# Loading the experts' rows from another queue, and reordering the end of the attention stage, in a fused attention, expert and feed-forward kernel

## What is computed

```python
# 1. linear attention: B, H, S, D = 2, 8, 768, 48
for t in range(S):
    kt, vt, rt = k[:, :, t], v[:, :, t], r[:, :, t]
    cur = einsum('bhd,bhe->bhde', u[None] * kt, vt)
    y[:, :, t] = einsum('bhd,bhde->bhe', rt, state + cur)
    state = w[None, :, :, None] * state + einsum('bhd,bhe->bhde', kt, vt)
# 2. experts: 1536 tokens of 384, 8 experts with 1024 hidden, at most 384 tokens each
logits = x @ w_gate                 # the best expert of each token
probs = softmax(logits)             # its probability weighs the result
h = maximum(disp @ w1[e], 0)        # disp: the expert's tokens, in order
out[i] = gate_w[i] * (h @ w2[e])[pos[i]]
# 3. feed-forward: 384 -> 2048 -> 384
h = x @ w_in
out = (h * clip(h + 3, 0, 6) / 6) @ w_out
```

## Time and profile before

| | |
|---|---|
| median of 3 runs | 525.84 us (524.63 to 528.38) |
| profiled execution | 524.35 us, its span 522.6 us |
| PE busy | 442.9 us, 85% of the span |
| DVE, ACT, POOL busy | 243.1, 209.2, 73.2 us |
| TensorE's granted clock, mean | 0.927 of full speed |
| transfers | 60.55 MB, mean 116 GB/s |

### The profile page before, as it was taken

One profiled execution on the slowest core, in us unless ns is written; L12 is line 12 of the kernel. 1 busy time (PEld: TensorE's weight loads), 2 busy tenths in 40 slices (PEclk: granted clock), 3 DMA queues, 4 the chain that ended last, 5 costly groups with the idle time before them and its releaser, 6 DMA issues.

```text
span 522.6 us, 7372 instructions
## 1 busy us (share of the span) xinstructions
PE 442.9 (85%) x2798; PEld 380.3 (73%) x2798; DVE 243.1 (47%) x491; ACT 209.2 (40%) x481; POOL 73.2 (14%) x85
## 2 busy tenths in 40 slices
PE   6878998894776839494949989999999999999994
PEld 3767887673776839494949867888878888788883
DVE  6837885642736336262718556222522333332222
ACT  2433677350615235252526465223433323422221
POOL 4727761301010101010101010000000000000000
PEclk9777999999696969698898999999999999999999
DMA  8698952426236270807165833000010000100001
GB/s 245 244 331 269 294 180 77 144 95 200 114 97 226 62 263 17 308 17 274 49 235 197 287 94 122 0 1 0 0 61 1 0 1 0 62 0 1 1 0 64
DMA packets 28681, 60.55 MB, mean 116 GB/s; under 512 B 2317, under 2 KB 19384, under 8 KB 28642
## 3 DMA queue, kind: packets, MB, share of 16 engines
q1 hardware_dynamic: 26850, 55.30, 31.7%
q0 software_dynamic: 1792, 4.73, 2.4%
HBM read 49.77 MB, written 11.04 MB: 116 GB/s over the span
## 4 chain that ended last, share of the span: by engine, by line
PE 67%; DMA 15%; issue 5%; DVE 5%; ACT 4%; POOL 3%; SPq 1%; POOLq 0%; DVEq 0%
PE ps L1472 19%; PE ps L1474 18%; PE ps L1473 18%; DMA raw<-in_w 9%; DMA y_dram<-y_sb,xg 4%; PE ps L1499 3%; PE ps L1379 1%; PE ps L1435 1%; PE ps L1410 1%; PE ps L1404 1%; DMA u_bc<-in_u_row 1%; POOL rk L608 1%; DVE w_lo L1062 1%; ACT w_hi L739 1%; POOL rku L612 1%
## 5 line engine op out<-in xcount | busy, mean ns | idle before, releaser
L1472 PE MATMUL ps<-x_hi,w_hi 128*128 128x256 f32 x144 | 47.2, 328 | 52.2 <-DVE h_lo L1170 50.4
L1205 DVE SCALAR_TENSOR_TENSOR u_sb<-t_sb,ps 128x512 f32<-128x512 f32 x48 | 33.0, 689 | 121.9 <-ACT t_sb L868 121.7
L868 ACT ACTIVATE t_sb<-ps,three 128x512 f32<-128x512 f32 x48 | 33.0, 689 | 117.3 <-PE ps L1474 117.2
L1472 PEld LDWEIGHTS ps<-x_hi,w_hi 128*128 128x128 f32 x144 | 33.1, 230 | 53.7 <-DVE h_lo L1170 51.6
L1062 DVE TENSOR_TENSOR w_lo<-raw,w_hi 128x384 fp32r<-128x384 f32 x64 | 34.5, 553 | 67.9 <-ACT w_hi L739 67.9
L1472 PE MATMUL ps<-h_hi,w_hi 128*128 128x512 f32 x144 | 57.5, 399 | 0.9 <-DVE h_lo L1211 0.8
L739 ACT ACTIVATE w_hi<-raw 128x384 fp32r<-128x384 f32 x64 | 32.1, 519 | 64.3 <-DMA raw<-in_w 64.3
L1474 PE MATMUL ps<-h_hi,w_lo 128*128 128x512 f32 x144 | 56.8, 395 | 0.0
L1472 PE MATMUL ps<-x_hi,win_hi 128*128 128x512 f32 x144 | 56.7, 394 | 0.0
L1473 PE MATMUL ps<-x_lo,win_hi 128*128 128x512 f32 x144 | 56.3, 391 | 0.0
L1474 PE MATMUL ps<-x_hi,win_lo 128*128 128x512 f32 x144 | 56.2, 390 | 0.0
(11 more groups left out here) (139 smaller groups left out, 802.6 us busy)
## 6 DMA issues: line engine op xcount, KB each, us to landing
raw<-in_w SPq DMA_DIRECT2D x16, 1536.0 KB, 9.7
tm_in<-in_krv_tm SPq DMA_DIRECT2D x12, 576.0 KB, 8.5
dm_in<-in_rk_dm SPq DMA_DIRECT2D x12, 448.0 KB, 10.9
xs_dram<-fill SPq DMA_DIRECT2D x1, 3088.0 KB, 10.4
raw_in<-in_w_in SPq DMA_DIRECT2D x8, 384.0 KB, 7.6
raw<-in_w_out SPq DMA_DIRECT2D x2, 1536.0 KB, 7.9
xg<-xs_dram SPq DMA_DIRECT2D x7, 386.0 KB, 3.2
x_stage<-y_dram SPq DMA_DIRECT2D x3, 768.0 KB, 4.8
```

Of the source, the lines that this page charges most:

```text
L868: nc.scalar.activation(t_sb[n % 2][:, :], ps[:, 3 + n % 3, :], ACT.Relu, bias=three[:, 0:1]).then_inc(t_done, 1)
L1205: nc.vector.scalar_tensor_tensor(out=u_sb[n % 2][:, :], in0=t_sb[n % 2][:, :], scalar=6.0, in1=ps[:, 3 + n % 3, :], op0=ALU.min, op1=ALU.m ...
L1472: mm(o, a_hi, b_hi, start=first, stop=False)
```

## The change

Six things, in the order of the diff:

- expert rows: load_xg moves from SP's queue to POOL's. load_xg(1) comes after the last send_x, load_xg(e+2) after send_y(e, 1); their waits are the same, with two for load_xg(1) written out. On SP nothing stands between raw1, raw2 and raw_in any more.
- the fill is two transfers of four experts each, behind load_tm(4) and load_tm(6); who waited for 16 now waits for 32.
- raw1(0) and raw2(0) are issued after load_tm(11), instead of in passes 7 and 9.
- ScalarE's tail: one eighth of w2 instead of four before the last moves, and another order of the rest.
- VectorE's tail: another order, and the wait for xg0 moves from first_x_lo to find_gate.
- TensorE's tail: another order; turn_x and logits of the last tile use bank 4 instead of 7, which takes a wait for state_ready in place of lg_moved, and half_turn_h waits for the last move_lg.

```diff
+    def turn_bank(n):
+        return 4 if n == NT - 1 else 7
...
@@ sync
-                    sp.wait_ge(fill_stored, 16)
+                    sp.wait_ge(fill_stored, 32)
...
-            def load_xg(e):
-                if e >= 2:
-                    for m in range(2):
-                        sp.wait_ge(y_sent[m], 16 * (e - 1))
-                sp.dma_start(xg[e % 2][:, :, :], slots_of[e, 0:MAIN, :].rearrange("(m p) n -> p m n", p=P)
-                             ).then_inc(ld_xg[e % 2], 16)
+            def clear_slots(g):
+                sp.wait_ge(s_fill, 2)
+                es = slice(E // 2 * g, E // 2 * (g + 1))
+                sp.dma_start(slots_of[es, 0:MAIN, :].rearrange("e (p m) n -> p e (m n)", m=2),
+                             fill[:, :, :].rearrange("p m n -> p (m n)").unsqueeze(1).to_broadcast([P, E // 2, 2 * ROW])
+                             ).then_inc(fill_stored, 16)
...
-                if n == 3:
-                    sp.wait_ge(s_fill, 2)
-                    sp.dma_start(slots_of[:, 0:MAIN, :] ...
-                if n == 7:
-                    load_raw1(0)
-                if n == 9:
-                    load_raw2(0)
+                if n in (4, 6):
+                    clear_slots((n - 4) // 2)
+            load_raw1(0)
+            load_raw2(0)
             load_half(0)
             load_in(0)
             load_half(1)
-            load_xg(1)
             for e in range(1, E):
                 load_raw1(e)
-                if e + 1 < E:
-                    load_xg(e + 1)
                 load_raw2(e)
                 load_in(e)
@@ gpsimd
+            def load_xg(e):
+                if e == 1:
+                    pool.wait_ge(x_sent_a, 16 * NA)
+                    pool.wait_ge(x_sent_b, 16 * NA)
+                else:
+                    for m in range(2):
+                        pool.wait_ge(y_sent[m], 16 * (e - 1))
+                pool.dma_start(xg[e % 2][:, :, :], slots_of[e, 0:MAIN, :].rearrange("(m p) n -> p m n", p=P)
+                               ).then_inc(ld_xg[e % 2], 16)
+            load_xg(1)
             for e in range(E):
                 for m in range(2):
                     send_y(e, m)
+                if e + 2 < E:
+                    load_xg(e + 2)
@@ scalar
-                if n == NT - 1:
-                    for f in range(4):
-                        w2_split_hi(0, f)
             weigh_v(NT - 1)
+            w2_split_hi(0, 0)
+            move_y(NT - 1)
+            move_xt(NT - 2)
             first_x_hi(0)
-            move_y(NT - 1)
+            move_lg(NT - 2)
             sum_exp(C - 2)
-            move_xt(NT - 2)
-            move_lg(NT - 2)
             move_xt(NT - 1)
             move_lg(NT - 1)
             sum_exp(C - 1)
-            for f in range(4, FC):
+            for f in range(1, FC):
                 w2_split_hi(0, f)
@@ vector
+            choose(C - 2)
             w1_split_lo(0, 0)
-            choose(C - 2)
-            dve.wait_ge(ld_xg0[0], 16)
-            first_x_lo(0)
             join(NT - 1)
             place(C - 2)
+            first_x_lo(0)
             w1_split_lo(0, 1)
...
             half_relu(0, 0)
+            dve.wait_ge(ld_xg0[0], 16)
             find_gate(0, slice(0, 1), 1)
@@ tensor
-                if n >= 1:
+                if turn_bank(n) == 4:
+                    pe.wait_ge(state_ready, PAIRS * (NT - B))
+                elif n >= 1:
                     pe.wait_ge(lg_moved, n)
...
             cum(C - 2)
-            half_first(0, 0, [(0, 0)])
             turn_y(NT - 1)
             logits(NT - 2)
             turn_x(NT - 1)
-            half_first(0, 0, [(0, 1)])
+            half_first(0, 0, [(0, 0)])
             logits(NT - 1)
-            half_first(0, 0, [(1, 0), (1, 1)])
+            half_first(0, 0, [(0, 1), (1, 0), (1, 1)])
             cum(C - 1)
             half_first(0, 0, [(2, 0), (2, 1)])
+            pe.wait_ge(lg_moved, NT)
             half_turn_h(0, 0)
```

More of the change, by code:

```diff
@@ L449, in _ @@
                 load_tm(n)
-                if n == 3:
-                    sp.wait_ge(s_fill, 2)
-                    sp.dma_start(slots_of[:, 0:MAIN, :].rearrange("e (p m) n -> p e (m n)", m=2),
-                                 fill[:, :, :].rearrange("p m n -> p (m n)").unsqueeze(1).to_broadcast([P, E, 2 * ROW])
-                                 ).then_inc(fill_stored, 16)
-                if n == 7:
-                    load_raw1(0)
-                if n == 9:
-                    load_raw2(0)
+                if n in (4, 6):
+                    clear_slots((n - 4) // 2)
+            load_raw1(0)
+            load_raw2(0)
             load_half(0)
@@ L619, in send_x @@
                 if n == 0:
-                    pool.wait_ge(fill_stored, 16)
+                    pool.wait_ge(fill_stored, 32)
                     pool.wait_ge(s_pool, 11)
@@ L715, in move_xt @@
                     act.wait_ge(lg_done, n)
-                nc.scalar.activation(x_tr[:, :, :], ps[:, 7, 0:D].rearrange("p (c t) -> p c t", t=P),
+                nc.scalar.activation(x_tr[:, :, :], ps[:, turn_bank(n), 0:D].rearrange("p (c t) -> p c t", t=P),
                                      ACT.Copy).then_inc(xt_moved, 1)
@@ L720, in move_lg @@
                 act.wait_ge(lg_done, n + 1)
-                nc.scalar.activation(lg_sb[:, n, :], ps[:, 7, D:D + E], ACT.Copy).then_inc(lg_moved, 1)
+                nc.scalar.activation(lg_sb[:, n, :], ps[:, turn_bank(n), D:D + E], ACT.Copy).then_inc(lg_moved, 1)
             def sum_exp(c):
@@ L1423, in turn_x @@
                 pe.wait_ge(x_ready, n + 1)
-                if n >= 1:
+                if turn_bank(n) == 4:
+                    pe.wait_ge(state_ready, PAIRS * (NT - B))
+                elif n >= 1:
                     pe.wait_ge(lg_moved, n)
                 for k in range(DC):
-                    i = nc.tensor.transpose(ps[:, 7, k * P:(k + 1) * P], x_stage[:, n, k * P:(k + 1) * P], ident[:, :])
+                    i = nc.tensor.transpose(ps[:, turn_bank(n), k * P:(k + 1) * P], x_stage[:, n, k * P:(k + 1) * P], ident[:, :])
                 i.then_inc(x_turned, 1)
@@ L1434, in logits @@
                 for k in range(DC):
-                    i = mm(ps[:, 7, D:D + E], x_tr[:, k, :], wg_sb[:, k, :], start=k == 0, stop=k == DC - 1)
+                    i = mm(ps[:, turn_bank(n), D:D + E], x_tr[:, k, :], wg_sb[:, k, :], start=k == 0, stop=k == DC - 1)
                 i.then_inc(lg_done, 1)
```

## The result

The changed kernel took 484.43 us (median of 4 runs, 476.33 to 487.84) against 526.59 before (4 runs, 524.63 to 528.38): a ratio of 0.911, 95% interval 0.8986 to 0.9234. It is faster, by 42 us at the medians; forecast were 479, range 459 to 500. The profiled execution took 485.81 us, with a span of 484.0.

The account below looks back on a forecast made before the run. It took SP's head-of-line wait for the scatters, which held back raw2, to bound the expert bodies. 524.35 - 45.9 (bodies) + 1.0 (attention stage) - 1.3 (tail) gave 478.2 us, 479 against the median, range 459 to 500.

Parts of the forecast that it names:

- The wait in SP's queue is what bounds the bodies, and raw2 arrives in time once it is free: Expert bodies: load_xg's wait for scatters delays raw2; moving it removes a stall of 8.4 us per body.
- xg is late next: Expert bodies: xg lands at T+11.9, T being the gated result; new stall 3.4 us (first body 1.5), body 20.9.
- The clock survives a stall of 3.4: Expert bodies: TensorE's clock keeps its upper level; from about 4 us of stall it costs some 2.2 per body.
- Front of the attention stage, -10.0: Attention stage up to scores(8): tm(4) ahead of the split fill brings scores(8) from 62.55 to 51.9; 10.0 us taken off.
- Its back, +11.0: Attention stage from pass 8: ScalarE waits 7.9 us for late raw1(0), then one low-clock pass adds 3.1.
- The tail, -1.3: End of the attention stage: one w2 split left, behind weigh_v(11), so tile 11's chain comes 1.3 us earlier.
- The sum: Whole kernel: 524.35 - 45.9 + 1.0 - 1.3 = 478.2 us for the profiled execution, 479 against the median.
- No new stall: Rival for the expert bodies: scatter and load land before T+8.5, giving 460 us, or 457; chance 0.22.
- A stall with low clock: Rival for the expert bodies: late POOL load, stall of 5 us plus 2.2 for low clock, 501 to 515; chance 0.18.
- Starvation of POOL's transfers: Rival for the expert bodies: xg's load starved behind SP's traffic, taking 14 us, total 550 us; chance 0.04.
- the queue is not what is paid for: Rival for SP's queue: the move saves only issue time, 2.2 us in all, total 522 to 525; chance 0.04.

Follow-up runs that it names:

- the queue alone: The kernel before with only the loads of the experts' rows moved from SP's queue to POOL: 484.47 us, ratio 0.9287.
- the early weights: The changed kernel with raw1(0) and raw2(0) issued in passes 7 and 9 again: 476.40 us, ratio 0.915.
- the fill alone: The kernel before with only the fill cut in two, behind tm(4) and tm(6): 517.26 us, ratio 0.9847.
- the row copy: Row numbers copied out of xg, freeing it earlier: changed kernel 461.14 us; kernel before, loads still on SP, 460.90 us; ratio 0.8821 each.

## Why the prediction was right, point by point

- **The wait in SP's queue is what bounds the bodies, and raw2 arrives in time once it is free.** Right: the stall of 50.4 us is gone, no matmul of the bodies waits for raw2. Body 1's slow start over w1's low part stayed, as reckoned.
- **xg is late next.** Right, and link by link: scatter 5.78 (5.5 was taken), pickup 0.53 (0.77), load 3.49 (4.3), landing at T+11.2 (T+11.9). The load's own 0.81 is the largest miss; POOL needs 0.76 us for it (149.69), less than for a scatter of half the rows, so the 1.08 added to 3.2 was too much. The other bodies but the first lie near: scatters 5.41 to 6.44, loads 3.31 to 3.72. Summed, TensorE waited 16.7 us, against 18.5 forecast.
- **The clock survives a stall of 3.4.** Wrong as a rule, and the largest miss of the sum. In the profiled execution it fell in four of six bodies, once behind a wait of 1.90 us and once behind 2.25, and held behind 2.81 and 3.33:

```profile
131.12 1.38 PE L1545 MATMUL ps<-ident,xg 128*128 128x128 f32 x6 [1.90 <-DMA xg<-xs_dram]
...
153.22 0.88 PE L1545 MATMUL ps<-ident,xg 128*128 128x128 f32 x6 [2.81 <-DMA xg<-xs_dram]
...
174.25 0.87 PE L1545 MATMUL ps<-ident,xg 128*128 128x128 f32 x6 [3.33 <-DMA xg<-xs_dram]
...
216.59 1.50 PE L1545 MATMUL ps<-ident,xg 128*128 128x128 f32 x6 [2.25 <-DMA xg<-xs_dram]
```

  TensorE's busy time is 19.3 in the four bodies where it fell and 17.7 in the two others, 1.6 us each, 6.4 in all. With 1.8 less stall that turns the forecast 125.4 into 130.0; 131.1 were measured. So the length of the stall alone doesn't say whether the clock falls: the six transposes took 0.88 and 0.87 us behind the longer waits and 1.38 and 1.50 behind the shortest. (Behind 3.15 and 3.28 us it fell a little later, during the second layer.) The two other profiles of these bodies say the same: behind 1.92 us it fell in one body of the queue alone, behind 3.17 it held in another; with the early weights it held in five of six, and those six took 125.7 us, the forecast 125.4. The clock is thus partly a matter of luck, and the profile that the sum is held against had a bad share of it.
- **Front of the attention stage, -10.0.** Right: scores of pass 8 at 53.41, -9.1 (52.65 to 54.53 in three other profiles with late weights); the fill alone gave 56.21 with weights in between.
- **Its back, +11.0.** Right in kind. ScalarE waited 5.7 instead of 7.9, since raw1 landed in 8.41 us and not in 10.3; but two passes ran at low clock, not one (it was down at 53.41 already, behind a wait of 1.46 us for rk_sc). From pass 8 to pass 11 it cost 12.3 (28.49 instead of 16.18). In the three other profiles ScalarE waited 6.3 to 6.4 us, only one of these passes began at low clock, as forecast, and the same stretch took 26.2 to 26.4: 10.1.
- **The tail, -1.3.** -1.6 in the changed kernel (81.90 to 105.51, 23.61) and alone.
- **The sum.** 478.2 for the profiled execution, 485.81 measured: +5.7 in the bodies, +0.9 and +1.3 in the attention stage, -0.3 in the tail. The rest is the same work: 234.1 us from the last body to the end, 234.0 before. In the bodies two errors have opposite signs, 1.8 us too much stall and a clock taken to hold.
- **The rivals.** No new stall (0.22) is what the row copy gives, at 107 us for six bodies, so its arithmetic was right for another kernel. A stall with low clock (0.18) came half true: its clock in some bodies, not its stall of 5 us. Starvation of POOL's transfers (0.04) didn't occur; the longest load landed in 6.7 us. That the queue is not what is paid for (0.04) is refuted as it was priced, 522 to 525 us: the queue alone gave 484.5. In its words it was nearer than its chance says, since the row copy gives more without any move.

That this kernel's own executions spread over 11 us fits a clock that falls in some bodies and not in others: their mean granted clocks are 0.98 at 476.33 us, 0.959 at 483.05, 0.960 at 485.81 and 0.951 at 487.84. Only one of them was profiled, so where in the kernel they differ is not shown.

## What to carry to other kernels

When an in-order queue stands at a wait, ask first what it waits for and whether that wait is needed, and only then where to put the instruction: copying 256 row numbers so that a buffer comes free a body earlier was worth more than the move to another queue (0.882 against 0.929), and made the move pointless here. A transfer put off past its neighbours still has its consumer at the old place in some engine's order; move the consumer too, or leave it early enough. Short stalls cost more than their length when the clock falls behind them, 1.6 us per body here, and whether it falls can change from one execution to the next; so give it a chance and a price, not a yes or no, and look at more than one profile before you call its effect measured.

## What the runs showed of the hardware

- A small transfer from POOL took 3 to 4 us longer beside a weight of 1536 KB from SP, and of two in a row the one that met the weight paid: with raw1 beside the scatter, 5.78 for the scatter and 3.49 for the load; with raw1 beside the load, 2.40 and 7.12.
- A plain load of 256 rows occupied POOL for 0.75 to 0.76 us in every body of the changed kernel, also at 124.38, where VectorE was 95% busy; a scatter of 128 rows took it 0.98 to 1.99 us, the longest at 120.22 beside VectorE's split of w1.
- The granted clock fell behind a wait of 2.25 us that followed 8.4 us of unbroken TensorE work at full clock (body 5 of the changed kernel), and held behind waits of 2.81 and 3.33 us in other bodies of the same execution.
